# Attention, two-expert routing and a cosine MLP in one kernel: expert weights split in other places and by other engines

## The reference

```python
# attention: 2 batches x 8 heads, 1152 keys, 576 pooled queries, head size 64
q_pool = q.reshape(B, H, S // 2, 2, D).mean(axis=3)
attn = softmax(q_pool @ k.T / sqrt(D));  x = (attn @ v) as [1152 tokens, 512]
# experts: 8, hidden 1024, two for each token
noisy = x @ w_gate + log1p(exp(x @ w_noise)) * noise
top2 = the two largest of noisy;  g = softmax over these two
out[token] = sum over its two experts e of g * (relu(x @ w1[e]) @ w2[e])
# last layer, hidden 2048
h = out @ w_in;  result = (h * cos(h)) @ w_out
```

## Time and profile before

| | us |
|---|---|
| median of 3 runs | 879.99 |
| lowest, highest | 877.95, 883.82 |
| profiled execution | 884.95 |
| its span | 883.2 |

### The profile page before, as it was taken

One profiled execution on the slowest core, in us unless ns is written; L12 is line 12 of the kernel. 1 busy time (PEld: TensorE's weight loads), 2 busy tenths in 40 slices (PEclk: granted clock), 3 DMA queues, 4 the chain that ended last, 5 costly groups with the idle time before them and its releaser, 6 DMA issues.

```text
span 883.2 us, 15491 instructions
## 1 busy us (share of the span) xinstructions
PE 852.7 (97%) x4894; PEld 757.8 (86%) x4895; DVE 494.6 (56%) x988; ACT 411.9 (47%) x753; POOL 420.3 (48%) x301
## 2 busy tenths in 40 slices
PE   7999999999999789998999999999998999999998
PEld 6999999999999678886887888888877889999997
DVE  6788778887888884231322222232234776676564
ACT  3677777777777531111112121121123665565544
POOL 8554455544554905768959959568314020000000
PEclk9999999999999989998999999999999999999999
DMA  5112111121150423887554645463316020100100
GB/s 137 55 42 81 41 40 40 42 78 40 40 163 0 145 100 124 294 283 251 190 178 144 220 146 179 140 194 131 131 36 227 1 71 1 37 1 0 37 1 36
DMA packets 51377, 90.50 MB, mean 102 GB/s; under 512 B 9360, under 2 KB 18576, under 8 KB 50832
## 3 DMA queue, kind: packets, MB, share of 16 engines
q1 hardware_dynamic: 40080, 65.29, 22.1%
q10 hardware_dynamic: 7904, 13.77, 4.8%
q0 software_dynamic: 3360, 11.01, 4.1%
HBM read 73.00 MB, written 17.06 MB: 102 GB/s over the span
## 4 chain that ended last, share of the span: by engine, by line
PE 80%; POOL 7%; DVE 5%; issue 3%; DMA 3%; ACT 2%; POOLq 0%; ACTq 0%; SPq 0%; DVEq 0%
PE ps L1531 8%; PE ps L1533 8%; PE ps L1532 8%; PE ps L1355 5%; PE ps L1385 4%; PE ps L1403 4%; PE ps L1386 4%; PE ps L1401 4%; PE ps L1402 4%; POOL W L604 4%; PE ps L1632 3%; PE ps L1631 3%; PE ps L1630 3%; PE ps L1617 3%; PE ps L1615 3%; PE ps L1616 3%
## 5 line engine op out<-in xcount | busy, mean ns | idle before, releaser
L604 POOL TENSOR_TENSOR W<-stage,W 128x2048 fp32r<-128x2048 f32 x36 | 165.3, 4594 | 2.7
L964 DVE TENSOR_REDUCE mx<-ps 128x1 f32<-128x384 f32 x225 | 119.6, 551 | 20.1 <-PE ps L1355 20.0
L976 DVE TENSOR_TENSOR pl__76<-ps,ph 128x576 fp32r<-128x576 f32 x144 | 108.0, 750 | 33.4 <-ACT ps L758 33.4
L753 ACT ACTIVATE ph<-ps 128x576 fp32r<-128x576 f32 x144 | 94.0, 653 | 62.2 <-PE ps L1386 61.1
L758 ACT ACTIVATE ps<-ps 128x576 f32<-128x576 f32 x144 | 93.3, 648 | 0.0
L1385 PE MATMUL ps<-qat,kt 128*128 128x288 f32 x288 | 84.9, 310 | 7.4 <-DVE pl__76 L976 6.4
L813 ACT CAST hh<-ps 128x512 fp32r<-128x512 f32 x50 | 26.9, 590 | 131.0 <-PE ps L1570 125.2
L1401 PE MATMUL ps<-ph,vs 128*65 128x288 f32 x288 | 86.6, 301 | 0.4 <-ACT ot L712 0.4
L1531 PE MATMUL ps<-W,xh 128*128 (+1 forms) x200 | 81.3, 407 | 5.2 <-POOL W L604 5.1
L1403 PE MATMUL ps<-ph,vs 128*65 128x288 f32 x288 | 85.4, 297 | 0.0
L1402 PE MATMUL ps<-pl__76,vs 128*65 128x288 f32 x288 | 85.2, 296 | 0.0
(11 more groups left out here) (206 smaller groups left out, 2019.4 us busy)
## 6 DMA issues: line engine op xcount, KB each, us to landing
stage<-in_moe_w_dram SPq DMA_DIRECT2D x32, 1024.0 KB
y_slots<-ys ACTq DMA_DIRECT2D x25, 256.0 KB
x_slots<-ring SPq DMA_DIRECT2D x22, 256.0 KB
xs<-x_slots ACTq DMA_DIRECT2D x22, 256.0 KB
kn<-in_k_dram SPq DMA_DIRECT2D x16, 288.0 KB, 3.3
vn<-in_v_dram SPq DMA_DIRECT2D x16, 288.0 KB, 2.8
stage<-in_moe_w_in_dram SPq DMA_DIRECT2D x4, 1024.0 KB
stage<-in_moe_w_out_dram SPq DMA_DIRECT2D x4, 1024.0 KB
```

The source lines that it names most:

```text
L604: pl.tensor_tensor(W[:, slot, 1, part], stage[:, j % 2, :], W[:, slot, 0, part].bitcast(F32), ALU.subtract).then_inc(w_ready, 1)
L964: ve.tensor_reduce(mx3[:, i:i + 1], ps[:, bank_of(hh, ("m", i)), 0:PIECE], AX_X, ALU.max).then_inc(m_ev, 1)
L976: ve.tensor_tensor(pl_[:, j % 3, :].rearrange("p (a n) -> p a n", a=2), ps[:, 2 * s_par(hh, j):2 * s_par(hh, j) + 2, 0:HQ], ph[:, j % 3, : ...
```

## The change

- GpSimd splits expert 0's four pieces in heads 13 to 16, one behind each head's work, which for that is written out behind a shorter loop. SyncE stages pieces 0 and 1 behind head 12's loads, piece 2 behind head 15's, piece 3 ahead of the store of the first batch, and pieces 0 and 1 of expert 1 right behind that store.
- The second batch of x is stored by SyncE, not by ScalarE.
- The one-hot rows of the second choice are made by ScalarE: Abs(place - p), then Relu(token - token * that), with a new buffer `away` and a negated copy of the token numbers (`minus_tok`). VectorE makes the first choice's rows only. TensorE's table matmuls wait for both.
- `rank_done` now counts ranks and counts apart, so that the selection doesn't wait for the counts.
- Expert 1: all four high parts by ScalarE (`high_w`), pieces 2 and 3 within tile 0; all four low parts by VectorE (`low_w`), two ahead of tile 0's relu and two within tile 0. GpSimd's 22 gathers into the ring now run without a split between them, and SyncE stages expert 1's pieces 2 and 3 ahead of the slots' stores.

```diff
...
+        minus_tok, at = place("minus_tok", at, [P, RT])
...
+        away, at = place("away", at, [P, RT, P])
...
-            with sp.Fori(1, NHEAD // 2) as p:
+            with sp.Fori(1, NHEAD // 2 - 2) as p:
                 load_head(p, 0)
                 load_head(p, 1)
...
+            pieces0, pieces1, pieces2 = expert_pieces(0), expert_pieces(1), expert_pieces(2)
+            for j in range(2):
+                stage_piece(0, j, pieces0[j])
             sp.wait_ge(zeroed, FILLS)
             nv = noise.rearrange("(b s) e -> b s e", b=B)
             for b in range(B):
                 sp.dma_start(nz[:, b * QC:(b + 1) * QC - 1, :],
                              nv[b, 0:(QC - 1) * P, :].rearrange("(c p) e -> p c e", p=P)).then_inc(noise_in, 16)
                 sp.dma_start(nz[0:QTAIL, (b + 1) * QC - 1, :], nv[b, (QC - 1) * P:SQ, :]).then_inc(noise_in, 16)
+            load_head(NHEAD // 2 - 2, 0)
+            load_head(NHEAD // 2 - 2, 1)
+            load_head(NHEAD // 2 - 1, 0)
+            stage_piece(0, 2, pieces0[2])
+            load_head(NHEAD // 2 - 1, 1)
+            stage_piece(0, 3, pieces0[3])
             sp.wait_ge(o_norm, H)
             for dst, src in x_parts(0):
                 sp.dma_start(dst, src).then_inc(x_stored, 16)
...
+            for j in range(2):
+                stage_piece(WPIECES, j, pieces1[j])
+            sp.wait_ge(o_norm, NHEAD)
+            for dst, src in x_parts(1):
+                sp.dma_start(dst, src).then_inc(x_stored, 16)
...
-            stage_set(0, expert_pieces(0))
-            for j, part in enumerate(expert_pieces(1)):
-                if j == 2:
-                    store_slots(*GATHERS[0])
-                stage_piece(WPIECES, j, part)
+            for j in range(2, WPIECES):
+                stage_piece(WPIECES, j, pieces1[j])
+            store_slots(*GATHERS[0])
             store_slots(*GATHERS[1])
-            for j, part in enumerate(expert_pieces(2)):
+            for j, part in enumerate(pieces2):
                 if j == 2:
                     store_slots(*GATHERS[2])
                 stage_piece(2 * WPIECES, j, part)
...
-            with pool.Fori(1, NHEAD // 2) as p:
+            with pool.Fori(1, NHEAD // 2 - 2) as p:
                 for par in range(2):
                     split_kq(p, par)
                     copy_k(2 * p + par - 1, 1 - par)
                     split_v(p - 1 + par, 1 - par)
+            for m in range(NHEAD - 4, NHEAD):
+                j, par = m - NHEAD + 4, m % 2
+                split_kq(m // 2, par)
+                copy_k(m - 1, 1 - par)
+                split_v((m - 1) // 2, 1 - par)
+                split_weights(0, j, 0, 16 * (j // 2 + 1))
...
-            gather_slots(*GATHERS[0])
-            split_weights(WPIECES, 0, 1, 16 * 3, high=False)
-            split_weights(WPIECES, 1, 1, 16 * 3, high=False)
-            gather_slots(*GATHERS[1])
-            pool.wait_ge(route_done, 1)
-            split_weights(WPIECES, 2, 1, 16 * 4)
-            split_weights(WPIECES, 3, 1, 16 * 4)
-            gather_slots(*GATHERS[2])
+            gather_slots(NDIRECT, SLOTS_T)
             with pool.Fori(1, E // 2) as ep:
...
-            for dst, src in x_parts(1):
-                act.dma_start(dst, src).then_inc(x_stored, 16)
+            def rows_of(b):
+                act.wait_ge(place_done, b + 1)
+                for c in range(QC):
+                    i = b * QC + c
+                    sc.activation(away[:, i, :], iota_p[:, :], ACT.Abs, scale=-1.0, bias=place_f[:, 0, 1, i:i + 1]
+                                  ).then_inc(away_done, 1)
+                for c in range(QC):
+                    i = b * QC + c
+                    act.wait_ge(away_done, b * QC + c + 1)
+                    last = sc.activation(row_of[:, 1, i, :], away[:, i, :], ACT.Relu, scale=minus_tok[:, i:i + 1],
+                                         bias=tok[:, i:i + 1])
+                last.then_inc(rows_done, 1)
...
+            def high_w(j):
+                act.wait_ge(stage_in[j % 2], 16 * (j // 2 + 3))
+                sc.copy(W[:, 1, 0, j * WPIECE:(j + 1) * WPIECE], stage[:, j % 2, :]).then_inc(wh_done, 1)
             soft_noise(1)
+            rows_of(0)
             act.wait_ge(gap_done, 2)
             sc.activation(e2[:, :], gap[:, :], ACT.Exp).then_inc(e2_done, 1)
             act.wait_ge(ot_done, NHEAD)
+            act.wait_ge(wh_done, WPIECES)
             for j in range(2):
-                act.wait_ge(wh_done, WPIECES + j)
-                act.wait_ge(stage_in[j], 16 * 3)
-                sc.copy(W[:, 1, 0, j * WPIECE:(j + 1) * WPIECE], stage[:, j, :]).then_inc(wh_done, 1)
+                high_w(j)
+            rows_of(1)
...
+                    act.wait_ge(route_done, 1)
+                    for j in range(2, WPIECES):
+                        high_w(j)
...
+                last.then_inc(place_done, 1)
+                dve.wait_ge(place_done, b + 1)
...
+            def rows_of(b):
                 for i in range(b * QC, (b + 1) * QC):
-                    last = ve.tensor_scalar(row_of[:, n, i, :], iota_p[:, :], place_f[:, 0, n, i:i + 1], tok[:, i:i + 1],
-                                            ALU.is_equal, ALU.mult)
-                return last
+                    ve.tensor_scalar(row_of[:, 0, i, :], iota_p[:, :], place_f[:, 0, 0, i:i + 1], tok[:, i:i + 1],
+                                     ALU.is_equal, ALU.mult)
...
+            dve.wait_ge(zeroed, FILLS)
+            ve.tensor_scalar(minus_tok[:, :], tok[:, :], -1.0, None, ALU.mult).then_inc(minus_done, 1)
...
             soft_max0(1)
-            dve.wait_ge(o_norm, NHEAD)
-            rows_of(0, 0)
             noisy_logits(1)
             top_two(1)
             top_index(1)
             members(1)
             running(1)
-            rows_of(0, 1)
+            dve.wait_ge(o_norm, NHEAD)
+            rows_of(0)
             dve.wait_ge(rank_done, 2)
             select_first(1, ranks_at(RANK1)[:, 0, :], sel1)
+            dve.wait_ge(rank_done, 3)
             then(ve.tensor_scalar(tiles_i[:, 0, :], ps[:, COUNTS, 0:E], 1.0, float(P - 1), ALU.max, ALU.add))
             then(ve.tensor_scalar(tiles_i[:, 1, :], tiles_i[:, 0, :], 7, None, ALU.logical_shift_right))
             then(ve.tensor_copy(tiles_f[:, :], tiles_i[:, 1, :]))
             then(ve.tensor_tensor_scan(cum[:, :], ones[:, 0:E], tiles_f[:, :], 0.0, ALU.mult, ALU.add))
             then(ve.tensor_tensor(tbase[:, :], cum[:, :], tiles_f[:, :], ALU.subtract))
             places(1, ranks_at(RANK1))
+            rows_of(1)
             for n in range(2):
-                rows_of(1, n)
                 last = ve.tensor_tensor(based[:, n, :, :], onehot[:, n, :, :],
                                         tbase[:, :].unsqueeze(2).to_broadcast([P, E, RT]), ALU.mult)
...
+            def low_w(j):
+                dve.wait_ge(wh_done, WPIECES + j + 1)
+                part = slice(j * WPIECE, (j + 1) * WPIECE)
+                ve.tensor_tensor(W[:, 1, 1, part], stage[:, j % 2, :], W[:, 1, 0, part].bitcast(F32), ALU.subtract
+                                 ).then_inc(w_ready, 1)
...
-            def tile_steps(t, left=3):
+            def tile_steps(t, left=3, first=False):
                 low_h(t)
+                if first:
+                    low_w(2)
                 if left >= 1:
                     relu_d(t + 1)
+                if first:
+                    low_w(3)
                 if left >= 2:
                     low_x(t + 2)
...
             route_gates()
+            low_w(0)
+            low_w(1)
             relu_d(0)
             low_x(1)
-            tile_steps(0)
+            tile_steps(0, first=True)
...
+                last.then_inc(rank_done, 1)
                 if b == 1:
-                    last = pe.matmul(ps[:, COUNTS, 0:E], ones[:, :], upto[:, :, RT - 1], start=True, stop=True)
-                last.then_inc(rank_done, 1)
+                    pe.matmul(ps[:, COUNTS, 0:E], ones[:, :], upto[:, :, RT - 1], start=True, stop=True
+                              ).then_inc(rank_done, 1)
...
             warm(WARM_R)
             pe.wait_ge(slot_of_done, 1)
+            pe.wait_ge(rows_done, 2)
             for n in range(2):
```

More of the change, by code:

```diff
@@ L174, in build @@
         sel_done = sem("sel_done")
+        place_done = sem("place_done")
+        away_done = sem("away_done")
+        minus_done = sem("minus_done")
+        rows_done = sem("rows_done")
         route_done = sem("route_done")
@@ L357, in build @@
         row_of, at = place("row_of", at, [P, 2, RT, P], F32R)
+        assert at <= AFTER_X + 13824
         tile_hot, at = place("tile_hot", at, [P, 2, RT, STW], F32R)
@@ L480, in expert_pieces @@
                         + pieces(w2[bass.ds(e, 1)].rearrange("o f d -> (o f) d"), 2))
+            pieces0, pieces1, pieces2 = expert_pieces(0), expert_pieces(1), expert_pieces(2)
+            for j in range(2):
+                stage_piece(0, j, pieces0[j])
```

(32 more changed lines are left out.)

1 line of the change is left out of this document (removed).

## The result

| | before | changed |
|---|---|---|
| median, us | 881.32 (877.95 to 883.82) | 868.62 (867.46 to 869.53) |
| ratio | | 0.9858, 95% interval 0.9819 to 0.9896 |
| profiled execution | 884.95 | 867.97 |
| its span | 883.2 | 866.2 |

What follows compares the result with a forecast made beforehand. TensorE, busy 97% of the span, bounds the kernel; only its idle or half-clock stretches count. 7.7 + 3.5 + 7.35 = 18.5 us off the profiled 884.95 gave 866.4, and 861.5 against the median, range 857.5 to 868.5.

Steps and rivals of the forecast that it cites:

- Step 1: Last head: expert 0's pieces split in heads 13 to 16 cost nothing there and save 7.7 us (bounds 6.7 to 8.1).
- E: Last head isn't freed, as VectorE's long instructions have another cause; only 10.8 us remain: 869.2; chance 0.05.
- F: Heads 13 to 16: GpSimd's pieces hold VectorE, up to 26 us for four, so 7.5 over before: 887.5; chance 0.04.
- Steps 2 and 3: Routing: SyncE's x store and ScalarE's second-choice rows let the table matmuls start 3.5 us sooner (bounds about 0 to 3.9).
- I take the full clock: Routing: the rank stop shrinks from 2.57 to 1.2 us, so ranks and selection were assumed at full clock.
- Rival B: Routing: clock falls all the same behind the shorter rank stop, table 2.3 us later: 863.8; chance 0.12.
- Step 4: Expert 1 on ScalarE and VectorE: nothing lost at tile 0, tile 6's interval becomes 12.25, saving 7.35 us (bounds 4.3 to 7.35).
- rival C: Tile 0 is overfilled: ScalarE stands before piece 3 while tile 1's relu waits, loss 3 to 7: about 866; chance 0.13.
- The rule against the change: Gathers beside VectorE's low pieces: second and third each wait for one, some 2 us later in all; first undisturbed; nothing feels it.
- Rival D: Tile 0: the lock holds the first gather too, until the first low piece is through, costing 1.3 us: 862.8; chance 0.06.

Runs made afterwards that it cites:

- heads-only one: Kernel before with only expert 0's four pieces split in heads 13 to 16: 872.84 us against 882.5, ratio 0.9896; a second execution on another chip took 877.15.
- kernel with that stop filled: Changed kernel plus 4 idle matmuls between tile 0's first selection and the ranks: 867.41 us, ratio 0.9842 to the kernel before.
- the fills above: Changed kernel with idle matmuls in rank stop, table, both, or both plus selection (4 or 1 ahead of the table): 867.41, 867.14, 868.64, 867.26, 867.10 us.
- third execution of before: Kernel before, unchanged, profiled a third time: 882.39 us, with a stop of 4.55 us and an interval of 19.09 us at tile 6.
- the one with the table filled: Changed kernel plus one idle matmul behind each five table matmuls, 3 in all, rank stop left: 867.14 us, ratio 0.9833 to the kernel before.
- later set that has both kernels: Changed kernel unchanged, profiled again on the same chip as the parts: 866.99 us, ratio 0.9839, 15.5 us under before there.
- stop and table filled: Changed kernel plus idle matmuls both in the rank stop and between the table matmuls: 868.64 us, ratio 0.9843 to the kernel before.

## Why the forecast was 7 us off

The 7.1 us between 861.5 and 868.62 are three parts: the changed kernel's profiled execution is 1.6 over the 866.4 that the sum gave it, 5.0 were subtracted to get from there to the median, and 0.6 lie between its profiled execution and its median.

A table of the stretches, in us, for the pair that the sum was made on (first profiled execution of each) and a second pair, in which before (882.39) is close to its median:

| stretch | forecast | first pair | second pair |
|---|---|---|---|
| start to head 15's turn of o (291.70) | 0 | -1.31 | -0.27 |
| to the last turn of o | -7.7 | -7.47 | -7.48 |
| to tile 0's first hidden matmul | -3.5 | -3.38 | -2.23 |
| to tile 0's turn of hidden rows | 0 | +1.61 | +1.65 |
| to tile 6's turn | -7.35 | -7.34 | -6.76 |
| to the end | 0 | +0.89 | -0.61 |
| sum | -18.5 | -17.0 | -15.7 |

**Step 1, heads 13 to 16: right.** The pieces cost nothing there. GpSimd splits one in each head (and is idle from 280.0 on, 281.3 on before's scale, not from 283; nothing hangs on that), and no row of TensorE before head 15's turn of o moves; the steps forecast for 297.65, 299.0, 300.55 and 301.85 came at 297.61, 298.93, 300.45 and 302.03 (the trace's times plus the 1.31 us of the start), and the first pair's stretch is 7.47 us shorter. Rivals E and F are out: with GpSimd's weight work moved away, in this kernel and in the heads-only one, the long VectorE instructions are gone.

**Steps 2 and 3, x and the rows: sizes right, the clock wrong.** Everything up to the table came as worked out: 1.18 us of stop for 1.2, ten rows on ScalarE in 3.5 us for 3.5, 3.38 us gained for 3.5. What failed is "I take the full clock". It held where I looked, behind the rank stop, and failed where I didn't: at tile 0's hidden part, 1.6 us in both profiled executions of the changed kernel. Rival B had the right loss in kind and the wrong place: it tied the fall to the stop, and the kernel with that stop filled falls all the same. And in a typical execution of before the selection is only partly slow (stretch 19.57 us and not 20.72), so there was less to gain than in the first one. The net term is 0.6 to 1.8 us in the profiles and 1.7 in the medians, where 3.5 stood. Why the clock falls there stays open.

**Step 4, expert 1: mechanism right, the term too large.** No loss at tile 0, neither from the two low pieces nor from ScalarE's copies (relu of tile 1 had 3.3 us to spare where I had 2.8), so rival C is out here; the fills above show how close it was. Expert 2's split starts at 376.59, behind the last gather and not behind tile 2: the gathers were over some 15 us later than worked out, one of them after 8.31 us of waiting for the ring. It was still in time, and tile 6's interval is 12.25 us. But 7.35 was the interval of one execution. Others lose 1.2, 6.0, 6.8 and 7.2 at the same place, and the medians put the term at 4.2 and 4.75.

**The step that cost most: the last one, from the execution to the median.** I saw that the profiled execution was 5 us over the median, sized each stall in it, and subtracted the whole sum from the median. Against the third execution of before (882.39) the first has 2.6 us more, and the table shows where: 1.0 in the start (half clock near 22 us), 1.2 in the selection, 0.5 at tile 6. The last two are stalls that the change takes away, so that part of the 5 us went with them and couldn't be subtracted once more; the first can fall on any execution, as it does on the one with the table filled. Another 1.3 us is the baseline: the median of three, 879.99, became 881.32 with a fourth execution, and other sets of before have 880.7 to 882.5. The changed kernel's profiled execution (867.97) lies inside its own timed ones. The forecast of its own time, 866.4, was 1.6 us off, as much as the clock at tile 0 cost; that the rest of the table adds up to nothing is in part luck (-1.31 at the start, +0.89 behind tile 6). The forecast against the median was 7.1 off. In the later set that has both kernels the gain is 15.5 us and not 12.7, so how much of the miss is this step isn't known better than to some 3 us. The range should have reached up for the case that the gain comes off the profiled execution's time alone: 866.4 with nothing lost, and the clock's and tile 0's rivals on top.

**The rule against the change.** As read from the earlier trace rows: gathers that start inside a low piece wait for its end, the first one doesn't. The changed kernel's GpSimd:

```profile
326.90 1.12 POOL L657 DMA_INDIRECT xd<-x_rows,tok_u  x1 [46.90 <-DVE tok_u L1298]
328.32 1.94 POOL L657 DMA_INDIRECT xd<-x_rows,tok_u  x1 [0.30 <-issue]
330.57 1.90 POOL L657 DMA_INDIRECT ring<-x_rows,tok_u  x1 [0.30 <-issue]
332.77 0.95 POOL L657 DMA_INDIRECT ring<-x_rows,tok_u  x1 [0.30 <-issue]
...
339.26 1.86 POOL L657 DMA_INDIRECT ring<-x_rows,tok_u  x1 [3.04 <-DMA ring<-x_rows,tok_u]
...
343.93 2.58 POOL L657 DMA_INDIRECT ring<-x_rows,tok_u  x1 [0.31 <-issue]
```

The low pieces end at 329.45 and 331.65; the second and third gathers end at 330.26 and 332.47, 0.81 and 0.82 us later. Two more start inside the later pieces, at 339.26 and 343.93 (pieces of 338.01 and 343.41), take 1.86 and 2.58 us and end 0.82 and 0.81 us behind them. None held TensorE: tile 1's turn came with no wait. Rival D is out, as the first gather took 1.12 us, exactly as before. Here trace and Trainium skill differ (SBUF — State Buffer, section "Who interferes with whom"): it infers that VectorE's `tensor_tensor` doesn't stall DMAs that GpSimd issues, and the trace shows indirect ones held for up to 1.6 us; the measurement decides.

## What to carry to other kernels

Size a stall in several executions before subtracting it from a median: a stop whose length depends on when transfers land was 0.95 us in one execution and over 4 in four (4.07 to 4.55), and a gain sized in one execution must come off that execution's own time. When a change removes idle time ahead of light matmuls, don't take full clock for the whole stretch behind it: look at every part of it, and in more than one execution. And work that one engine does in a hurry at a stage's end can go into the slots that it idles in each round before (9 us in each head here, for pieces of 6.8); where that work held up another engine, as here, all of that loss comes back (7.5 us).

## What was not expected of the hardware

- The granted clock fell to its lower level with TensorE stopped for no more than 0.36 us in the 8 us before (326 to 330 us, both profiled executions of the changed kernel; again with the rank stop filled, and later and longer with stop and table filled), behind short matmuls of selection and table; and it stayed up behind a stop of 2.56 us in one execution and fell behind the same stop in another of the same kernel, on another chip.
- An indirect gather of GpSimd, normally 0.95 us, took 1.94, 1.90, 1.86 and 2.58 us when it started inside a 128x2048 VectorE subtraction with two SBUF inputs, each time ending 0.81 to 0.82 us behind it; one that had started 0.26 us before such a subtraction took 1.12, as without it.
- The tiny `minus_tok` product (10 columns) took 0.88 us at 16.75, ending at 17.63, 0.04 us behind a GpSimd instruction that started at 15.99 and took 1.60: it looks like the stall of the last head in small, at no cost there (under 0.2 us had been forecast).
- A whole execution has tiles of 12.25 or of 12.29 us. Both values occur for the same kernel (before: 12.25, 12.29, 12.25); over 25 tiles that is 1 us, as much as the fills could bring. Profiled executions on one chip have either value, so the chip alone doesn't decide it.
